# A two-layer expert stage: turning the hidden activations by DMA and VectorE squares instead of TensorE transposes

## The reference

```python
kv = np.einsum('bhsd,bhse->bhde', k, v)
out = np.einsum('bhsd,bhde->bhse', q, kv)
x = out / sqrt(mean(out * out) + 1e-06) * g_norm          # 8 x 576 tokens, 512 features
...
logits = x @ w_gate + modality_bias[modality_id]          # 8 experts
e_idx = np.argmax(logits, axis=1)
gate_w = softmax(logits)[e_idx]
for e in range(E):
    h = np.maximum(x[mask] @ w1[e], 0.0)                  # 512 -> 1024
    out[mask] = gate_w[mask, None] * (h @ w2[e])          # 1024 -> 512
...
out = (sigmoid(x @ w_gate) * (x @ w_val)) @ w_out         # 512 -> 1536 -> 512
```

## Time and profile before

| | |
|---|---|
| median of three runs | 1538.6 us |
| the profiled execution's own time | 1532.99 us |
| its span in the trace | 1530.8 us |
| mean granted clock of TensorE, of full speed | 0.958 |
| TensorE matmul busy | 1416.6 us, 93% of the span |
| VectorE busy | 863.6 us, 56% |
| ScalarE busy | 435.1 us, 28% |
| share of the chain that ended last: TensorE | 82% |

### The profile page before, as it was taken

One profiled execution on the slowest core, in us unless ns is written; L12 is line 12 of the kernel. 1 busy time (PEld: TensorE's weight loads), 2 busy tenths in 40 slices (PEclk: granted clock), 3 DMA queues, 4 the chain that ended last, 5 costly groups with the idle time before them and its releaser, 6 DMA issues.

```text
span 1530.8 us, 25386 instructions
## 1 busy us (share of the span) xinstructions
PE 1416.6 (93%) x8566; PEld 1167.5 (76%) x8567; DVE 863.6 (56%) x1430; ACT 435.1 (28%) x766; POOL 287.4 (19%) x364
## 2 busy tenths in 40 slices
PE   4776379999999999988999999999999999999997
PEld 4665268878888888876778888888888888888885
DVE  3566665476636665346685556655575555755541
ACT  4555022222222222234432213321242222421121
POOL 0055324334333443321101001100011000110011
PEclk9677589999999999999999999999999999999998
DMA  9782244355524454429978443174424634144320
GB/s 340 295 309 107 79 111 140 97 169 158 150 80 144 146 159 136 102 53 329 325 260 231 154 159 143 65 210 149 152 113 137 185 144 147 72 172 144 145 76 28
DMA packets 113485, 241.67 MB, mean 158 GB/s; under 512 B 17655, under 2 KB 62711, under 8 KB 107264
## 3 DMA queue, kind: packets, MB, share of 16 engines
q1 hardware_dynamic: 75296, 199.41, 39.0%
q0 software_dynamic: 11200, 29.69, 5.8%
q10 hardware_dynamic: 26912, 11.51, 2.9%
HBM read 179.44 MB, written 51.73 MB: 151 GB/s over the span
## 4 chain that ended last, share of the span: by engine, by line
PE 82%; DVE 6%; DMA 4%; issue 3%; ACT 2%; SPq 1%; POOL 0%; ACTq 0%; DVEq 0%; POOLq 0%
PE ps L1523 29%; PE ps L1503 17%; PE ps L1472 14%; PE ps L1450 13%; PE ps L1459 2%; PE ps L1373 2%; PE ps L1386 2%; DMA graw<-in_moe_w_val 1%; PE ps L1350 1%; DMA mixes<-mix 1%; PE ps L1493 1%; DMA vt<-in_v 1%; DMA xs<-x_rows,seat_x 0%; ACT qp L716 0%; DVE mix L1213 0%
## 5 line engine op out<-in xcount | busy, mean ns | idle before, releaser
L1523 PE MATMUL ps<-a_hi,st 128*128 128x512 f32 x1344 | 421.4, 389 | 0.9 <-DVE u L1295 0.9
L1523 PEld LDWEIGHTS ps<-a_hi,st 128*128 128x128 f32 x1344 | 252.4, 188 | 54.1 <-DVE a_lo L1256 1.5
L1503 PE MATMUL ps<-wo,shi 128*128 128x512 f32 x864 | 269.8, 394 | 5.5 <-DVE slo L1265 4.7
L1523 PE MATMUL ps<-a_lo,st 128*128 128x512 f32 x672 | 261.4, 389 | 0.0
L1450 PE MATMUL ps<-ew,xhi 128*128 x640 | 202.3, 397 | 18.6 <-DVE xlo L1125 17.2
L1472 PE MATMUL ps<-ew,hhi 128*128 x640 | 197.1, 389 | 1.3 <-DVE hlo L1141 1.3
L1503 PEld LDWEIGHTS ps<-wo,shi 128*128 128x128 f32 x864 | 163.1, 189 | 43.9 <-issue 3.5
L661 POOL DMA_INDIRECT out<-ot,out_tok x36 | 35.9, 997 | 717.7 <-ACT ot L815 711.9
L1503 PE MATMUL ps<-wo,slo 128*128 128x512 f32 x432 | 170.5, 395 | 0.0
L1450 PEld LDWEIGHTS ps<-ew,xhi 128*128 128x128 f32 x640 | 117.9, 189 | 42.7 <-issue 19.9
L1523 PEld LDWEIGHTS ps<-a_lo,st 128*128 128x128 f32 x672 | 126.1, 188 | 26.1
(11 more groups left out here) (223 smaller groups left out, 1841.0 us busy)
## 6 DMA issues: line engine op xcount, KB each, us to landing
st<-mixes SPq DMA_DIRECT2D x48, 1792.0 KB, 7.2
raw<-in_moe_w SPq DMA_DIRECT2D x64, 512.0 KB, 3.6
mixes<-mix SPq DMA_DIRECT2D x24, 512.0 KB, 8.3
xg<-xs ACTq DMA_DIRECT2D x158, 64.0 KB, 2.2
kt<-in_k SPq DMA_DIRECT2D x8, 1152.0 KB, 9.4
vt<-in_v SPq DMA_DIRECT2D x8, 1152.0 KB, 12.9
qt<-in_q SPq DMA_DIRECT2D x8, 1152.0 KB, 9.0
mixes<-gv SPq DMA_DIRECT2D x12, 768.0 KB, 6.8
```

Of the source, the lines that this page charges most:

```text
L1503: last = mm(ps[:, 4 + m, :], s[:, rows], wo[f // 2][:, w, f % 2], start=(f == 0 and w == 0 and s is shi[slot]), stop=(f == GC - 1 and s is ...
L1523: last = mm(bank_of(f, idx), st[f % 2][:, at:at + 128], x[:, idx, k, :], start=(k == 0 and w == 0 and x is a_hi), stop=(k == 1 and w == 1))
```

## The change

Each half of h is copied out of PSUM as before, and then brought by two DMAs of 128 KB each, issued on ScalarE's queue, into a new buffer `hq`, in which each group of 32 partitions holds one quarter (256) of the features and every partition holds four tokens. VectorE turns the 32x32 squares of `hq` into `ht` (two instructions), reading every eighth element (32 bytes apart). ScalarE copies the high part from `ht` instead of PSUM, VectorE the low part from `ht`. The rows of w2 are read in another order to fit. The TensorE transposes go. The PSUM banks they used become a second set for h, and y gets a second bank. `xt` has one buffer instead of two. The four matmuls on zeros ahead of the stage become 16 smaller ones, and the zero tile goes.

```diff
-    w2_v = w2.rearrange("e (c i p) d -> e c p i d", i=2, p=128)
+    w2_v = w2.rearrange("e (p c i) d -> e c p i d", p=128, i=2)
...
             def h_of(t):
                 for f in range(2):
                     if f == 0:
-                        wait(act, pe_hT, 2 * t.n)
+                        wait(act, hlo_made, 2 * t.n)
                     act.wait_ge(pe_h, 2 * t.n + f + 1)
-                    nc.scalar.activation(h[:, 512 * f:512 * f + 512], ps[:, 1 + f, :], ACT.Relu).then_inc(h_made, 1)
+                    nc.scalar.activation(h[:, 512 * f:512 * f + 512], ps[:, 1 + 2 * t.p + f, :], ACT.Relu).then_inc(h_made, 1)
+                    if f == 0:
+                        wait(act, ht_made, 2 * t.n)
+                    act.wait_ge(h_made, 2 * t.n + f + 1)
+                    for g in (2 * f, 2 * f + 1):
+                        act.dma_start(hq[32 * g:32 * g + 32], h[:, 256 * g:256 * g + 256]).then_inc(h_in, 16)
+
+            def hhi_of(t):
                 for f in range(2):
                     if f == 0:
                         wait(act, pe_y, t.n)
-                    act.wait_ge(pe_hT, 2 * t.n + f + 1)
-                    nc.scalar.copy(hhi[:, 512 * f:512 * f + 512], ps[:, 3 + f, :]).then_inc(hhi_made, 1)
+                    act.wait_ge(ht_made, 2 * t.n + f + 1)
+                    nc.scalar.copy(hhi[:, 512 * f:512 * f + 512], ht[:, 4 * f:4 * f + 4, :].rearrange("p x t -> p (x t)")).then_inc(hhi_made, 1)

             def tile_step(i, c, has_before):
                 use(Tile(i, c + 1), xhi_of)
                 use(Tile(i, c), h_of)
                 use(Tile(i, c + 2), load_x)
+                use(Tile(i, c), hhi_of)
...
             def x_turned(t):
                 dve.wait_ge(x_in[t.p], 64 * (t.half + 1))
-                wait(dve, xhi_made, t.n - 1)
+                wait(dve, xhi_made, t.n)
+                wait(dve, xlo_made, t.n)
...
+            def h_turned(t):
+                dve.wait_ge(h_in, 64 * (t.n + 1))
+                for f in range(2):
+                    nc.vector.transpose(ht[:, 4 * f:4 * f + 4, :].rearrange("p x (t r) -> p t x r", r=32),
+                                        hq[:].rearrange("p t (i x) -> p t x i", x=FC)[:, :, 4 * f:4 * f + 4, :]).then_inc(ht_made, 1)
...
                 if has_before:
                     use(Tile(i, c), split_rest)
+                use(Tile(i, c), h_turned)
+                if has_before:
                     use(Tile(i, c - 1), y_of)
                 use(Tile(i, c), hlo_of)
                 use(Tile(i, c + 2), x_turned)
...
             def up(t, e):
-                wait(pe, h_made, 2 * t.n)
+                wait(pe, h_made, 2 * (t.n - 1))
...
-            def h_transposed(t):
-                wait(pe, hlo_made, 2 * t.n)
-                for f in range(2):
-                    pe.wait_ge(h_made, 2 * t.n + f + 1)
-                    for c in range(4):
-                        n = 4 * f + c
-                        last = nc.tensor.transpose(ps[:, 3 + f, 128 * c:128 * c + 128], h[:, 128 * n:128 * n + 128], ident[:])
-                    last.then_inc(pe_hT, 1)
...
             def tile_step(i, c, has_before):
                 use(Tile(i, c), lambda t: up(t, expert(t)))
                 if has_before:
                     use(Tile(i, c - 1), lambda t: down(t, expert(t)))
-                use(Tile(i, c), h_transposed)
```

More of the change, by code:

```diff
@@ L344, in moe_program @@
         xt_made = sem("xt_made")
-        pe_h, pe_hT, pe_y = (sem(n) for n in ("pe_h", "pe_hT", "pe_y"))
+        pe_h, pe_y = sem("pe_h"), sem("pe_y")
+        h_in, ht_made = sem("h_in"), sem("ht_made")
         xhi_made, h_made, hhi_made = (sem(n) for n in ("xhi_made", "h_made", "hhi_made"))
-        xlo_made, hlo_made, y_made = (sem(n) for n in ("xlo_made", "hlo_made", "y_made"))
+        xlo_made, hlo_made = sem("xlo_made"), sem("hlo_made")
+        y_made = [sem(f"y_made{n}") for n in range(2)]
         graw_in, wraw_in, ghi_made, glo_made = (sem(n) for n in ("graw_in", "wraw_in", "ghi_made", "glo_made"))
@@ L620, in scatter @@
             def scatter(t):
-                when(y_made, t.n + 1)
+                when(y_made[t.p], t.half + 1)
                 nc.gpsimd.indirect_dma_start(
@@ L758, in xhi_of @@
                 act.wait_ge(xt_made, t.n + 1)
-                nc.scalar.copy(xhi[:, t.p], xt[:, t.p].rearrange("p c t -> p (c t)")).then_inc(xhi_made, 1)
+                nc.scalar.copy(xhi[:, t.p], xt[:].rearrange("p c t -> p (c t)")).then_inc(xhi_made, 1)
             def h_of(t):
@@ L882, in _ @@
             nc.vector.memset(g_tab[:, 2:4], 1.0)
-            nc.vector.memset(zero[:], 0.0)
             nc.vector.memset(ones[:], 1.0)
@@ L1124, in xlo_of @@
                 dve.wait_ge(xhi_made, t.n + 1)
-                nc.vector.tensor_tensor(xlo[:, t.p], xt[:, t.p].rearrange("p c t -> p (c t)"), xhi[:, t.p].bitcast(F32), ALU.subtract).then_inc(xlo_made, 1)
+                nc.vector.tensor_tensor(xlo[:, t.p], xt[:].rearrange("p c t -> p (c t)"), xhi[:, t.p].bitcast(F32), ALU.subtract).then_inc(xlo_made, 1)
             def y_of(t):
@@ L1140, in hlo_of @@
                     cols = slice(512 * f, 512 * f + 512)
-                    nc.vector.tensor_tensor(hlo[:, cols], ps[:, 3 + f, :], hhi[:, cols].bitcast(F32), ALU.subtract).then_inc(hlo_made, 1)
+                    nc.vector.tensor_tensor(hlo[:, cols], ht[:, 4 * f:4 * f + 4, :].rearrange("p x t -> p (x t)"), hhi[:, cols].bitcast(F32), ALU.subtract).then_inc(hlo_made, 1)
                 done, goal = split_range(t.n)
@@ L1428, in _ @@
             mm(ps[:, 6, 64:65 + NT], turn_f[:], list_f[:], start=True, stop=True).then_inc(pe_turned, 1)
-            for n in range(4):
-                mm(ps[:, 7, :], ident[:], zero[:], start=True, stop=True)
+            for n in range(16):
+                mm(ps[:, 7, 0:128], ident[:], ident[:], start=True, stop=True)
             def expert(t):
@@ L1449, in up @@
                             first, end = c == 0 and x is xhi and part == 0, c == DC - 1 and x is xlo
-                            last = mm(ps[:, 1 + f, :], x[:, t.p, rows], weights(e, c, part, cols), start=first, stop=end)
+                            last = mm(ps[:, 1 + 2 * t.p + f, :], x[:, t.p, rows], weights(e, c, part, cols), start=first, stop=end)
                     last.then_inc(pe_h, 1)
-            def h_transposed(t):
-                wait(pe, hlo_made, 2 * t.n)
-                for f in range(2):
-                    pe.wait_ge(h_made, 2 * t.n + f + 1)
-                    for c in range(4):
-                        n = 4 * f + c
-                        last = nc.tensor.transpose(ps[:, 3 + f, 128 * c:128 * c + 128], h[:, 128 * n:128 * n + 128], ident[:])
-                    last.then_inc(pe_hT, 1)
             def down(t, e):
-                wait(pe, y_made, t.n)
+                wait(pe, y_made[t.p], t.half)
                 pe.wait_ge(w_split, UNITS * e + UNITS)
@@ L1471, in down @@
                         first, end = c == 0 and x is hhi and part == 0, c == FC - 1 and x is hlo
-                        last = mm(ps[:, 5, :], x[:, rows], weights(e, DC + c // 2, part, cols), start=first, stop=end)
+                        last = mm(ps[:, 5 + t.p, :], x[:, rows], weights(e, DC + c // 2, part, cols), start=first, stop=end)
                 last.then_inc(pe_y, 1)
```

18 lines of the change are left out of this document (10 added, 8 removed).

## The result

The kernel became slower: a median of 1706.05 us (1701.06 to 1707.24, 4 runs) against 1538.15 us (1536.18 to 1540.94, 4 runs) of the kernel before on the same chip. The ratio is 1.1084, 95% interval 1.1055 to 1.1113. The forecast was 1674 us, in a range from 1625 to 1740. The profiled execution took 1701.06 us, with a span of 1699.0 us.

What follows compares the result with a forecast made beforehand. TensorE bounds the kernel before; afterwards a ring through VectorE's and ScalarE's written order does. Stage 128 us more, first tile 4, last four tiles 3: 135 us on 1538.6 gives 1674 us, range 1625 to 1740.

Steps and rivals of the forecast that it cites:

- The ring through split, x_turned, xhi and relu: Expert stage, written order of VectorE and ScalarE, hlo to hlo: 16.5 us with a split, 12.2 without; TensorE needs 10.93.
- 1, split: VectorE, from hlo end to the end of the weight split: 5.34 us, unchanged by the change.
- 2, x turned and xhi: After the split, x turned on VectorE 0.62 us, then its high part on ScalarE 0.66 us; unchanged.
- 4, two issues: ScalarE issues two DMA copies of h after the first relu, ahead of the second: 1.25 us.
- 6, two more issues and landing: After the second relu, last issue starts 0.66 us later, landing 2.5 us (bounds 2.1 and 4.7): together 3.15 us.
- 7, turns: Two VectorE instructions turning h with strided reads: 1.10 us each, 2.2 us for both, bounds 1.41 and 2.2.
- 8, y and hlo: VectorE after the turns: two small copies about 0.21 us, y 0.75 us, then hlo; together 2.16 us.
- Nothing is given back later: Behind the expert stage: the gated layer starts when the last `down` has ended, so the stage's loss stays.
- The clock: Rival: TensorE standing still drops its clock to 1.2 GHz, steps 20.5 us, 1880 us if it stayed; 6%.
- Hidden: Rival: turning h fits under TensorE's `up` and `down`, 10.93 us a tile, stage gains 34 us: 1505 us; 4%.
- Low bounds: Rival: h copies land in 2.2 us and turns take 0.7 us, steps 15.4 and 11.1 us: 1631 us; 20%.
- Colliding transfers: Rival: h copies share DMA engines with weight loads, landing 4.7 us instead of 2.5, 86 us more: 1760 us; 12%.

Runs made afterwards that it cites:

- the last run: Changed kernel with relus ahead of xhi, split behind turning of x, neighbouring reads with matching w2 rows, raw weights of experts 1 to 7 cut to one eighth: 1518.5 us.
- the light loads: Changed kernel with raw weight loads of experts 1 to 7 cut from 512 KB to 64 KB each: 1688.6 us.
- the run with the split behind: Changed kernel with VectorE's weight split moved after the turning of x instead of ahead of it: 1631.0 us.

## Why the prediction was right, and where it was off

**The bound.** Right. The ring through split, x_turned, xhi and relu set the pace; TensorE waited for xlo ahead of `up` (30 us in all) and for hlo ahead of `down` (125 us). One reordered line on ScalarE took 113 us back. What the prediction did not list is the ring of h itself, from relu to hlo and back to the relu. It took up its terms, the way of h alone, only as a time that must fit under TensorE's 10.9 us. That did not touch the forecast, since the longer ring hid it, but it is what the kernel ran into once the relus were moved ahead.

**The terms.** For the step shown above, by the prediction's numbers: 1, split, 4.90 us (forecast 5.34; the register loads showed 0.58 us where 1.06 was taken over from before). 2, x turned and xhi, 0.63 and 0.65 (0.62 and 0.66). 3, relu, 0.50 (0.50). 4, two issues, 1.29 (1.25). 5, second relu, 0.72 (0.65). 6, two more issues and landing, 613.28 - 609.07 = 4.21 (3.15). 7, turns, 2.07 (2.2). 8, y and hlo, 1.95 (2.16). The sum is 16.92, as measured; the forecast's was 16.5. The mis-sized term is 6: the landing was taken as 2.5 us by a line between 64 KB and 512 KB, took 3.6 in this step, and has a median of 3.4 in the changed kernel, 3.2 with the weight loads cut. The terms taken too high, 1, 7 and 8, hid most of that: 1.06 us too little against 0.78 too much. That the sum came so near this step was in part luck.

**The total.** The stage from first to last hlo took 832.87 - 213.49 = 619.4 us, 155.8 more than before; the forecast was 128 + 3. The first tile's extra, the first hlo at 213.49 instead of 207.07, is 6.4 us (4). What lies behind the last hlo took 866.1 us instead of 860.2, 6 us more (0). Sum: 155.8 + 6.4 + 5.9 = 168 us, forecast 135.

**Nothing is given back later: not refuted.** In this trace 6 us more lie behind the last hlo. Of these, 4.2 lie ahead of the first matmul of the gated layer (14.6 us after the last hlo starts, 10.5 before the change) and 1.8 behind it. The gated layer began at a low clock:

```profile
847.48 0.76 PE L1503 MATMUL ps<-yhi,gv 128*128 128x512 f32 x1 [6.44 <-DVE gv L1215]
848.04 0.63 PE L1503 MATMUL ps<-ylo,gv 128*128 128x512 f32 x1
848.47 1.05 PE L1503 MATMUL ps<-yhi,gv 128*128 128x512 f32 x2
849.32 0.63 PE L1503 MATMUL ps<-ylo,gv 128*128 128x512 f32 x1
```

Three of them take 1.28 us (849.32 - 848.04), the pace of the lower level, 1.2 GHz, after 6.44 us of standing still. Before the change the same place had 3.69 us of idle time and no fall. But that was one execution. The control that changes only the PSUM sets runs the same gated layer behind the same idle time, and there the clock did fall:

```profile
679.79 0.77 PE L1494 MATMUL ps<-yhi,gv 128*128 128x512 f32 x1 [3.69 <-DVE gv L1196]
680.36 0.63 PE L1494 MATMUL ps<-ylo,gv 128*128 128x512 f32 x1
680.78 1.05 PE L1494 MATMUL ps<-yhi,gv 128*128 128x512 f32 x2
681.64 0.63 PE L1494 MATMUL ps<-ylo,gv 128*128 128x512 f32 x1
```

Its part behind the last hlo took 867.5 us, 7.3 more than in the trace of the kernel before. So the 6 us are no more than two executions of the same code differ by, and can't be put down to the change.

**The clock.** This rival came true in part and cost little. Windows of the changed kernel (same columns as above):

```profile
250.00:800.00 550.00, 430.86 (x1639) 336.79 (x1639) 289.20 (x412) 100.95 (x172) 178.67 (x207) 0.90 0.48 132
```

The granted clock was 0.90 in the stage, 1.00 before. A fall stood behind the 3.99 us of idle time ahead of 600.00, none behind the 3.51 us ahead of 616.92. In the step shown the slower matmuls from 600.00 to 604.8 ended in a `down` that still was done 7 us before y needed it: the slack the prediction named held. From first to last hlo, no wait of VectorE or ScalarE is put down to a matmul. The gap without a fall in the earlier trace rows, which the prediction set against this rival, was a weak argument: the same gap was followed by a fall in the control above. The rule cited from the Trainium skill (TensorE: Matmul & The Clock Gate, "HAM oscillation"), that bursts between waits for DMA bring the clock down again and again, agrees with this trace in kind (0.90, and matmuls at the pace of the lower level), but the 1880 us that the prediction worked out for a clock that stays low did not come.

**The other rivals.** Hidden: refuted for the order as written, since steps took 17.2 us; borne out in the last run, where the order was mended and the loads were light: 34 us less from first to last hlo. Low bounds: the stride does cost 0.4 us a turn, as line 968 had said, so only the landing could have brought it, and it went the other way. Colliding transfers: 0.6 us in a step with a split, some 17 us in all by the light loads, not 86. The argument against it (the last h issue comes after the load has landed) did not quite hold, since weight loads now took a median of 4.8 us and not 3.6: in the step shown the load issued at 605.44 landed at 610.63, 1 us after the last h issue. The move of the split shows what the argument was worth: beside the loads, a copy took 6.8 us.

**The fabric rule.** The Trainium skill (DMA: Bandwidth & Descriptors, "Where 436 GB/s comes from") has copies within SBUF bound by a fabric of 435 GB/s. The estimate from that figure, a copy of 128 KB only 0.15 us slower than one of 64 KB, is not what these runs show: 3.4 us against 2.2, or 3.2 with most of the other traffic gone. The measurement decides. The x copies of 64 KB stand four in a row too and land after 2.2 us, and the fastest of the 160 h copies needed 2.9, so the row alone is not the reason; what makes the doubled copy a full microsecond slower was not measured by itself and stays open.

## What to carry to other kernels

When an engine that sets the pace is relieved, write down the rings that close through the program order of the other engines, add one of them up from the trace, and compare it with the new pace; a sum from rows of the old trace came within 4% of the median step here, 16.5 against 17.2 us, in part because errors cancelled, and the landing of a copy of a size that the trace does not have is the term to give a wide range. Do it again for the order that you would mend it to: behind the first ring stood a second one, closed by two buffers that share memory. Ask of every move what the moved work was covering, and what transfers it triggers at its new place. A transpose of 0.88 us on the bound engine is cheap against the 8.3 us of terms 4 to 7, unless these are off the ring.

## What was not expected of the hardware

- SBUF copies of 128 KB in pieces of 1 KB land 3.4 us (median) after issue, with a minimum of 2.9; those of 64 KB in pieces of 512 bytes, issued in the same way, took 2.2 us before the change and 2.6 after it.
- Beside 512 KB loads the same copies needed 6.8 us in the step shown of the run with the split behind.
- A 32x32-square turn of 128x512 float32 takes 1.10 us when it reads every eighth element and 0.69 us when it reads neighbours.
- TensorE's clock was at the lower level behind idle times of 3.99 and 6.44 us, and at the higher behind one of 3.51 us in the next step. Behind an idle time of 3.69 us at the same place of the program it was at the higher level in one execution and at the lower in another. An idle time does not tell by itself whether it falls.
